# Attention, routed experts and a Fourier mixer on one core: a second output bank during routing, batch 0's routing as single steps in pairs 6 and 7, the first expert's weights and the rows loaded at other places

## The reference, cut to what matters

```python
logits = np.einsum('bsd,de->bse', x, w_gate)             # 8 experts
local_gate = 1.0 / (1.0 + np.exp(-(x @ w_local)))
...
e = fresh_e if s == 0 or local_gate[b, s] < 0.5 else prev_e   # the token's expert, in order of the tokens
out[b, s] = p[e] * (np.maximum(x[b, s] @ w1[e], 0.0) @ w2[e])  # w1[e] 512x1024, w2[e] 1024x512
```

## Time and profile before

| | |
|---|---|
| median of 3 runs | 712.22 us (703.8 to 712.31) |
| the profiled execution's own time | 705.74 us |
| its span | 703.9 us |
| mean granted clock of PE | 0.951 of full speed |
| PE / DVE / ACT / POOL busy, share of the span | 91% / 53% / 40% / 18% |
| attention, to the last values | 0 to 146 us |
| experts, to the last second layer | 146 to 354.4 us |
| Fourier stage and dense layer | 354.4 to 703.9 us |

### The profile page before, as it was taken

One profiled execution on the slowest core, in us unless ns is written; L12 is line 12 of the kernel. 1 busy time (PEld: TensorE's weight loads), 2 busy tenths in 40 slices (PEclk: granted clock), 3 DMA queues, 4 the chain that ended last, 5 costly groups with the idle time before them and its releaser, 6 DMA issues.

```text
span 703.9 us, 11369 instructions
## 1 busy us (share of the span) xinstructions
PE 639.0 (91%) x3276; PEld 541.2 (77%) x3277; DVE 376.4 (53%) x953; ACT 278.6 (40%) x601; POOL 124.1 (18%) x147
## 2 busy tenths in 40 slices
PE   4899977899788979999789999999999999999994
PEld 3898967787567767887553468998899899989993
DVE  4888577716854715255235176664544454454442
ACT  3688653714252613144001154445444334444430
POOL 5756431800300001000000041102000040000001
PEclk9999997959899989999897999999999999999997
DMA  7867422763775535301350333000100010000001
GB/s 160 166 146 159 100 61 87 278 244 94 266 260 195 169 129 176 130 30 60 134 194 1 140 106 114 1 1 1 45 1 1 0 45 0 0 28 16 0 0 45
DMA packets 63362, 66.56 MB, mean 95 GB/s; under 512 B 44064, under 2 KB 44192, under 8 KB 62304
## 3 DMA queue, kind: packets, MB, share of 16 engines
q1 hardware_dynamic: 58976, 54.57, 25.7%
q0 software_dynamic: 2480, 8.15, 3.3%
q10 hardware_dynamic: 1872, 3.44, 1.5%
HBM read 52.19 MB, written 13.95 MB: 94 GB/s over the span
## 4 chain that ended last, share of the span: by engine, by line
PE 68%; DVE 11%; issue 8%; DMA 6%; ACT 3%; SPq 2%; DVEq 1%; POOL 1%; ACTq 1%; POOLq 0%
PE bank L1678 19%; PE bank L1665 17%; PE bank L1558 8%; PE bank L1533 4%; DVE parts L1122 4%; DMA mid<-sorted_x 3%; PE bank L1404 2%; PE bank L1605 2%; PE bank L1449 2%; PE bank L1413 1%; PE bank L1424 1%; PE bank L1618 1%; PE bank L1629 1%; ACT arena L661 1%; PE bank L1638 1%
## 5 line engine op out<-in xcount | busy, mean ns | idle before, releaser
L1122 DVE TENSOR_TENSOR parts<-arena,parts 128x512 fp32r<-128x512 f32 (+1 forms) x148 | 108.4, 765 | 86.0 <-ACT parts L806 78.3
L1665 PE MATMUL bank<-parts 128*128 128x384 f32 x768 | 146.1, 338 | 2.4 <-DVE parts L1122 2.4
L1678 PE MATMUL bank<-parts 128*128 128x512 f32 x576 | 143.8, 394 | 0.5 <-DVE parts L1337 0.3
L1665 PEld LDWEIGHTS bank<-parts 128*128 128x128 f32 x768 | 135.4, 188 | 7.4 <-DVE parts L1122 3.1
L1678 PEld LDWEIGHTS bank<-parts 128*128 128x128 f32 x576 | 106.8, 188 | 21.4 <-DVE mid L1305 1.1
L1558 PE MATMUL bank<-parts 128*128 128x512 f32 x312 | 79.8, 414 | 10.2 <-issue 5.5
L1533 PE MATMUL bank<-parts 128*128 128x512 f32 x312 | 80.6, 416 | 1.7 <-DVE parts L1122 1.7
L1558 PEld LDWEIGHTS bank<-parts 128*128 128x128 f32 x312 | 61.3, 200 | 25.4 <-issue 6.7
L1533 PEld LDWEIGHTS bank<-parts 128*128 128x128 f32 x312 | 61.6, 202 | 14.9 <-DVE parts L1122 1.3
L806 ACT ACTIVATE parts<-arena 128x512 fp32r<-128x512 f32 x64 | 40.4, 631 | 82.3 <-PE bank L1678 82.3
L1122 DVE TENSOR_TENSOR parts<-bank,parts 128x512 fp32r<-128x512 f32 (+1 forms) x56 | 35.0, 647 | 43.9 <-ACT parts L796 23.5
(11 more groups left out here) (197 smaller groups left out, 804.7 us busy)
## 6 DMA issues: line engine op xcount, KB each, us to landing
mid<-in_moe_w SPq DMA_DIRECT2D x20, 512.0 KB, 5.7
arena<-in_moe_w SPq DMA_DIRECT2D x20, 512.0 KB, 5.2
sorted_x<-zero_row SPq DMA_DIRECT2D x16, 258.0 KB, 5.8
arena<-in_moe_w_ch SPq DMA_DIRECT2D x2, 2048.0 KB, 7.6
arena<-in_moe_w_ch SPq DMA_DIRECT2D x4, 1024.0 KB, 10.0
mid<-sorted_x ACTq DMA_DIRECT2D x13, 258.0 KB, 2.9
arena<-in_k SPq DMA_DIRECT2D x16, 192.0 KB, 3.2
arena<-in_q SPq DMA_DIRECT2D x16, 192.0 KB, 4.1
```

Source lines behind the costliest of these rows:

```text
L1122: return dve.tensor_tensor(out, whole, upper.bitcast(F32), ALU.subtract)
L1665: last = pe.matmul(bank[2 + f % 2][:, 0:GN], w[:, f % 2, r], x[:, par, c, :], start=(c == 0 and w is m1_hi and x is cT_hi), stop=(c == DC ...
L1678: last = pe.matmul(bank[4 + t][:, :], x[:, f % 2, r], w[:, f % 2, :], start=(f == 0 and x is g_hi and w is m2_hi), stop=(f == MC - 1 and w ...
```

## The change: what it does

- Outputs alternate between banks 5 and 6 in all pairs; scores have two banks instead of three (0, 1), and the bank set free (2) takes the turned gate tiles. Logits, codes and counts lie in columns beside the outputs, so PE waits for an output to be read (`bank_free`) and DVE for values (`av_ps`) ahead of them.
- A gate tile is turned a step earlier: `turn_gate` 0 to 5 in pair 4, with five of its six `logits`.
- `choose`, `share_first`, `write_steps`, `gate` and `positions` are cut into functions of one to three instructions. `link` becomes `settle` (wait for the last one marked) and `mark`, and the functions are called after the probabilities, the masks and the outputs of a step (`after_probs`, `after_masks`, `after_outputs`). Batch 0's table is written in the last step of pair 6, not in its step 1. Batch 1's parts stand in tile 1 (places) and tile 2 (table).
- SP clears batch 0's rows first, loads the first w1 behind the table and the first w2 still during pair 7, then the rows of tiles 0 to 3; batch 1's clearing stands ahead of `next_expert(3)`, and the rows of tiles 4 and 5 ahead of the loop of `next_expert`.
- The first w1 is split by ACT in steps 3 to 5 of pair 7 and subtracted by DVE, not POOL; the first w2 is split right behind.
- Sorted rows lie where batch 0's tiles of x were (`xa[:, n, :]`): one place each for tiles 0 to 3, then two in turn. ACT loads the rows of tile n + 2 at the start of tile n, from n = 4 on.
- The loops over the later tiles on PE, DVE and ACT take two tiles a round.

The core of the diff:

```diff
+        def xs(n):
+            return xa[:, n, :]
...
-        S_BANK, T_BANK, O_BANK, Q_BANK = bank[0:3], bank[3:5], bank[5:7], bank[7]
-        G_BANK = bank[6]
-        def out_bank(i, t):
-            return bank[5] if isinstance(i, int) and i >= HP else O_BANK[t % 2]
+        S_BANK, T_BANK, O_BANK, Q_BANK = bank[0:2], bank[3:5], bank[5:7], bank[7]
+        G_BANK = bank[2]
...
-            sp.wait_ge(vsum_ok, PAIRS)
+            sp.wait_ge(zero_set, 1)
+            clear_rows(0)
             sp.wait_ge(table_ok, 1)
             e = expert(0)
+            sp.wait_ge(vsum_ok, PAIRS)
             for c in range(DC):
                 load_w1(e, c, w1_first[c])
-            sp.wait_ge(zero_set, 1)
-            clear_rows(0)
+            sp.wait_ge(qk_ps, 3 * PAIRS)
+            sp.wait_ge(s_ps, ST * (PAIRS - 1))
+            for c in range(DC):
+                if c == DC - 1:
+                    sp.wait_ge(s_ps, ST * PAIRS)
+                load_w2(e, c, w2_first[c])
             sp.wait_ge(scattered[0], 16 * ST)
             sp.wait_ge(zeroed[0], 16 * E)
-            row = sp.value_load(table_i[0:1, T_ROW:T_ROW + 1], min_val=0, max_val=E * REGION - 1)
-            sp.dma_start(xs, sorted_x[bass.ds(row * P, P), :]).then_inc(xs_in, 16)
-            sp.wait_ge(av_ps, ST * PAIRS + SIX)
-            for c in range(DC):
-                load_w2(e, c)
-            for n in range(1, ROUND):
+            for n in range(ROUND):
+                load_rows(n, xs_first[n])
+            for n in range(1, ROUND - 1):
                 next_expert(n)
+            clear_rows(1)
+            next_expert(ROUND - 1)
             sp.wait_ge(table_ok, 2)
-            clear_rows(1)
+            sp.wait_ge(scattered[1], 16 * ST)
+            sp.wait_ge(zeroed[1], 16 * E)
+            for n in (ROUND, ROUND + 1):
+                load_rows(n, xs_in)
+                sp.wait_ge(xs_in, 16 * (n - 1))
             with sp.Fori(ROUND, SLOTS) as n:
                 next_expert(n)
...
                 pool.wait_ge(pos_ok, b + 1)
+                pool.wait_ge(gate_ok, b + 1)
...
             scatter(0)
-            for c in range(DC):
-                pool.wait_ge(w1_hi_ok, DC + c + 1)
-                pool.tensor_tensor(w1_lo[:, c, :], w1_raw[:, c, :], w1_hi[:, c, :].bitcast(F32), ALU.subtract).then_inc(w1_lo_ok, 1)
             scatter(1)
...
-                        if last_pair and 1 <= t <= DC:
-                            act.wait_ge(w1_first[t - 1], 16)
-                            upper_w1(t - 1)
+                        if last_pair and t >= ROUND - 1:
+                            upper_first(w1_hi, w1_raw, w1_first, w1_hi_ok, t - ROUND + 1)
...
-            def load_rows(n):
-                act.wait_ge(x_ps, n)
-                act.wait_ge(meta_in, n)
+            def load_rows(n, at):
+                act.wait_ge(x_ps, n - 1)
+                act.wait_ge(meta_in, n - 1)
+                act.wait_ge(xs_in, 16 * (n - 2))
...
+            def after_masks(i, t):
+                if t and (i, t) in GATE_SUM or i == HP + 1 and t >= 2:
+                    dve.wait_ge(av_ps, ST * i + t + SIX)
+                if (i, t) in GATE_SUM:
+                    fetch_logits(GATE_SUM[i, t])
...
+                elif (i, t) == (HP + 2, 1):
+                    cap_tiles()
+                    own_exponential(0)
...
             def tile(n, at):
...
                 with dve.If(0 < following):
                     split_w1(following)
-                if not first:
+                if known == 1:
+                    fetch_counts(1)
+                    own_places(1)
+                    sum_places(1)
+                    write_places(1)
+                    sum_exponentials(1)
...
+                elif known == 2:
+                    run_tiles(1)
...
+                    write_steps(1)
+                if known != 0:
                     output(n - 1)
...
-            with pe.Fori(ROUND, SLOTS) as n:
-                with pe.If(n < used):
-                    first_layer(n)
-                    turn_rows(n + 1)
+            with pe.Fori(0, STEPS[1] // 2) as pairs:
+                for par in range(2):
+                    n = 2 * pairs + (ROUND + par)
+                    with pe.If(n < used):
+                        first_layer(n)
+                        turn_rows(n + 1, ROUND + 1 - par)
```

592 lines of the change are left out of this document (381 added, 211 removed).

## The result

| | before | after |
|---|---|---|
| median of 4 runs, us | 709.84 (703.8 to 712.31) | 683.73 (678.7 to 685.22) |
| span of the profiled execution, us | 703.9 | 683.3 |
| ratio of the times | | 0.963 (0.954 to 0.972) |
| end of attention (last values) | 146.0 | 137.7 |
| from there to `second_layer(1)` | 49.8 | 39.8 |

The forecast was 680 us; the profiled execution took 685.22. The median before now has one run more than the one shown above. The five stretches of the table hold the whole gain, 20.6 us of span, and nothing changed behind the experts.

What follows compares the result with a forecast made beforehand. Undisturbed attention was taken as bound by PE, with routing pairs, PE's waits and its half clock adding time. From 705.74 us, -15.1 - 12.3 + 11.3 - 9.4 = -25.5 gave 680 us, range 660 to 705.

Steps and rivals of the forecast that it cites:

- Pairs 4 to 6: Attention with routing: pair 4 grows 1.5 us, pair 5 takes 16.0, pair 6 takes 13.9, set by DVE's work.
- Pair 7: Last pair of attention: 14.4 us instead of 18.5, values ending at 130.9 instead of 146.0, -15.1 for attention.
- less 2.8 for the last 5.7 us at half clock: Term of pair 7: PE's clock no longer falls at its end, 2.8 us won.
- rival 2: Clock stays at half from pair 7 into the first expert as before; 691 us, chance 0.16.
- for which I take 1.0 because the load is issued before the pair begins: Term of pair 7: ACT standing at the first quarter of w1, +1.0 us, bounds 0 and 5.7.
- Attention to `second_layer(1)`: From the last values to that layer, 49.8 us before: less half clock and waits for hidden rows, -12.3, bounds -16 and -2.
- clock 1.00 where 140 to 160 has 0.5 now: Sign for the profile after: PE's clock at full in the stretch that ran at half before.
- The new wait: Before first layer 4, third w1 behind batch 1's rows in SP's queue: PE waits 8.5 us, +11.3 in all, bounds 0 and 16.
- I am wrong if ... the idle time before first layer 4 is under 3 us: Sign against the forecast: PE idle there under 3 us, where about 8 us were expected.
- Later tiles: Expert tiles: row waits of 1.89 and 3.67, slow work of 2.8 and 1.0 at the loop's end go; -9.4, bounds -3 and -12.
- The Trainium skill's rule: Transfers from different engines share 16 DMA engines; if the first w1 quarter's landing doubled from 5.7 us, some 686; not added.
- The sum: Whole kernel: -25.5 against the profiled 705.74 us, so 680 us; the forecast's own range 670 to 690, chance 0.45.

Runs made afterwards that it cites:

- chained: Changed kernel with the steps of batch 0's table back in one place, step 1 of pair 6, each waiting for the one before; ratio 0.970 to the kernel before.
- clear_late: Changed kernel with SP clearing batch 0's rows behind the load of the first w1, as before the change; ratio 0.967 to the kernel before.
- scatter_late: row4_first's kernel with POOL's scatter of batch 0 behind the first output of pair 7; one execution 674.29 us, timed again at 0.960 of the kernel before.
- row4_first: Changed kernel with store_first's edit and SP loading rows of tile 4, then the third w1, then rows of tile 5; ratio 0.956 to the kernel before.
- w1_store: Changed kernel with the edits of w1_ahead and store_first together; ratio 0.962 to the kernel before.
- w1_ahead: Changed kernel with the third expert's w1 ahead of the rows of tiles 4 and 5 in SP's queue; one execution, 681.25 us.
- store_first: Changed kernel with POOL storing the first output ahead of its wait for batch 1's table; one execution, 688.26 us.
- rows_one_ahead: Changed kernel with ACT's load of the rows of tile n + 2 at the end of tile n instead of its start; one execution, 682.95 us.

## Why the prediction was right, point by point

**Pairs 4 to 6: right.** Predicted starts of pairs 5, 6 and 7 were 86.6, 102.6 and 116.5; measured 86.50, 103.21 and 116.95. The start of pair 5 agrees partly by luck: pair 4 began 0.75 us later than before and grew by 0.7 us for its two gate steps, not by 1.5. Pair 5 took 16.7 us (16.0 predicted) and pair 6 13.7 (13.9), with DVE busy 4.97 of 5 us in 110 to 115 and PE 3.52, as the reading of pair 6 as set by DVE has it; chained shows that the spreading is what made pair 6 short. One thing the prediction did not read: before the change the clock had fallen in pair 6 as well, to 0.64 in 115 to 120, at the wait of 4.51 us, and was at 0.68 while PE was busy behind it, and that time came back too:

```profile
120.00:125.00 5.00, 5.00 (x30) 4.83 (x29) 4.04 (x19) 2.02 (x6) 2.55 (x4) 0.68 0.78 286
```

**Pair 7: two terms that were mis-sized.** 14.4 us were predicted, 20.7 measured. The larger miss is "less 2.8 for the last 5.7 us at half clock": the clock fell again, earlier, and 10.7 us of the pair ran at half speed, about 5.3 us (worked out from these rows). The prediction had charged such a fall to rival 2 instead, and that rival came in part: the clock stayed at 0.50 to 150, not to 160. The smaller one is "for which I take 1.0 because the load is issued before the pair begins": w1 was issued 2.15 us into the pair, some 1.8 of it because SP's clearing transfers stood in front of the table's read (clear_late issues w1 1.0 us behind the table) and the rest because the table was written only 0.6 us before the pair. The wait was inside its bounds (0 to 5.7), at 2.17 for ACT and 1.81 for PE, 0.8 over the 1.0. That the wait brought the clock down is not shown: in scatter_late, without it, the clock fell a window later (130 to 135 instead of 125 to 130) and the pair took 17.0 us, still 2.6 over the forecast; in row4_first and w1_store, with larger waits in PE, it was back at 0.97 and 1.00 in 130 to 135.

**Attention to `second_layer(1)`: nearly right.** -10.0 instead of -12.3. The 3.40 and 1.07 us waits and the slow first layer went, as predicted; the half clock at 138 to 150 was kept, of which 1.6 us had been allowed for; "clock 1.00 where 140 to 160 has 0.5 now" came only from 150 on.

**The new wait: right in time, wrong in place.** w1 was issued 18.7 us behind `second_layer(1)` (predicted 19.1), and first layer 4 began 29.5 behind it (predicted 28.5). But PE did not stand 8.5 us in front of first layer 4. It stood 1.53 there, and 1.52 and 4.44 before, for rows and for DVE; by the prediction's own sign ("I am wrong if ... the idle time before first layer 4 is under 3 us") this part was wrong in its mechanism, and the time agrees partly by luck. The step that was missing is POOL's: the prediction said that the table is written later "where DVE has slack" and did not ask who waits for that table. POOL did, with the first output's store in its queue. Since w1 was the last of three things that were late by about the same, the sum did not notice; w1_ahead and store_first, which each take away one, gave 1.6 us and nothing. One link of the forecast's own chain was another, too: the scatter landed at T + 8.7, as forecast (T + 9), but the rows waited for SP's eight clearing transfers, landed at T + 9.8, which the chain did not hold. No run moves them.

**Later tiles: right, a little larger.** From T to the end of the experts the change gave -2.2 us where +1.9 was predicted: the row waits are gone, as rows_one_ahead confirms for one of them from the other side, the loop's end gave 1.8 instead of 1.0 (no run shows that two tiles a round did it), and the slow second layer, put behind first layer 4, lies in front of it.

**The Trainium skill's rule.** The doubled landing of the first w1 quarter did not happen: 5.88 us beside the clearing and the scatter, against a median of 5.7 before. A landing more than doubled where two loads followed each other in one queue, the rows behind w1 (6.9 us instead of 2.68).

**The sum.** Attention ended 6.8 us later than forecast and the stretch to `second_layer(1)` gave 2.3 less, while the tiles from T on gave 4.1 more. So the 5 us between 680 and 685.22 are what is left of larger misses on either side, and that much of the agreement is luck.

## What to carry to other kernels

When a value is moved to be written later, list every engine that waits for it, those far off the critical path too: the store of an output behind a table left PE idle for 4.44 us, where the transfer that had been watched left it idle for 1.53. When several things become late by about the same amount at one place, curing one shows little; order the transfers by when they are needed, the small one that is needed first in front, and cure them together. When a forecast counts on the clock staying up, give that term bounds of its own: here it missed by 5.3 us where the wait beside it missed by 0.8. Compare the stretch that no edit touches first: it alone differed by 5.6 us between profiles.

## What the runs showed of the hardware that was not expected

- PE's clock stood at half at the end of attention or fell to it within 6 us of that in all thirteen profiles after the change; it fell at a wait of 1.81 us in the change, and in scatter_late with no single wait of over 0.5 us in the 15 us before. It stayed at 0.50 through 5 us windows in which PE was busy all the time (145 to 150 after the change).
- DVE was held 2.9 to 3.65 us with no releaser in the profile but "remote", in eight of thirteen profiles, ending 1.1 to 1.4 us behind POOL's scatter in seven. It was missing from two of six profiles with the same code, from the one with 64 increments in front of DVE's program and from the two with a later scatter; what brings it is open.
- The rows of a tile took 2.68 us to land by themselves and 6.9 behind 2 MB of w1 in the same queue.
- Executions of the same attention code ended it between 136.9 and 141.9 us, and the same code behind the experts took 343.8 to 349.4 us.
